# Nine expert blocks of the first two batches computed between the attention tiles of the last two, with a routing of their own

## The reference, cut to what matters

```python
# q, k, v: (4, 8, 576, 64); d_model 512; 8 experts, hidden size 1024
scores = q @ k.T / 8;  keep the 32 largest of each row;  softmax;  attn = p @ v
x = attn, heads side by side                                   # (4, 576, 512)
logits = x @ w_gate;  local = sigmoid(x @ w_local)
for b, s:                                                      # in order of s
    e = argmax(logits[b, s]) if s == 0 or local[b, s] < 0.5 else previous e
    p = softmax(logits[b, s])
    out[b, s] = p[e] * (relu(x[b, s] @ w1[e]) @ w2[e])         # a gated expert
X = real(fft(fft(out, axis=1), axis=2))
u = out + X;  result = u + relu(norm(u) @ w_ch1) @ w_ch2
```

## Time and profile before

| | us |
|---|---|
| median of 3 runs | 1572.55 (1571.76 to 1573.14) |
| the profiled execution | 1576.68 |
| its span, first to last instruction | 1574.9 |
| TensorE busy | 1410.1 (90%) |
| VectorE busy | 1075.2 (68%) |
| GpSimd busy | 635.8 (40%) |
| ScalarE busy | 605.1 (38%) |

### The profile page before, as it was taken

The page is one execution under the profiler, slowest core; times in us unless marked ns, Lnnn a source line. Parts: engine busy times, 40 slices in busy tenths (PEclk is TensorE's granted clock), DMA queues, the critical chain, the costliest instruction groups (busy, mean ns, idle before and its releaser), DMA issues. The chain is left out here.

```text
span 1574.9 us, 24676 instructions
## 1 busy us (share of the span) xinstructions
PE 1410.1 (90%) x8488; PEld 1205.7 (77%) x8488; DVE 1075.2 (68%) x2132; ACT 605.1 (38%) x1469; POOL 635.8 (40%) x520
## 2 busy tenths in 40 slices
PE   6888888888889889984889999968999999999998
PEld 5777777776767677773779999963678789989997
DVE  8999999999999999997435555546646422422222
ACT  3555545555555554541324444422322221321110
POOL 4666666666866666651344444332112100000000
PEclk9989989999899997995999999985899999999999
DMA  9101011111101110102142726443321111411111
GB/s 322 42 23 31 24 32 32 32 32 32 32 8 32 32 29 28 69 1 80 42 156 70 257 68 244 174 174 126 107 97 56 46 40 53 137 52 41 40 41 61
DMA packets 67938, 117.95 MB, mean 75 GB/s; under 512 B 27827, under 2 KB 27956, under 8 KB 67842
## 3 DMA queue, kind: packets, MB, share of 16 engines
q1 hardware_dynamic: 57306, 87.17, 16.9%
q0 software_dynamic: 9728, 28.06, 5.1%
q10 hardware_dynamic: 808, 1.48, 0.3%
HBM read 88.36 MB, written 31.99 MB: 76 GB/s over the span
## 5 line engine op out<-in xcount | busy, mean ns | idle before, releaser
L332 POOL TENSOR_SCALAR keep<-s_sb,top 128x576 f32<-128x576 f32 x142 | 244.8, 1724 | 223.7 <-DVE top L356 223.7
L356 DVE MAX8 top<-w_sb 128x8 f32<-128x576 f32 x432 | 303.9, 743 | 0.0
L227 PEld LDWEIGHTS ps_o<-v_sb,eT 128*128 128x128 f32 (+1 forms) x1440 | 197.5, 202 | 37.4 <-issue 26.3
L227 PE MATMUL ps_o<-v_sb,eT 128*128 128x74 f32 (+3 forms) x1440 | 221.5, 294 | 0.0
L1393 DVE SCALAR_TENSOR_TENSOR h_lo<-ps_ch,h_hi 128x384 fp32r<-128x384 f32 x96 | 53.5, 557 | 241.9 <-ACT h_hi L1244 241.8
L358 DVE MATCH_REPLACE8 w_sb<-top,w_sb 128x576 f32<-128x576 f32 x288 | 211.1, 739 | 0.0
L336 POOL TENSOR_TENSOR e_sb<-e_sb,keep 128x576 f32<-128x576 f32 x142 | 200.1, 1409 | 21.4 <-POOL keep L332 0.6
L199 PE MATMUL ps_t<-ident,e_sb 128*128 128x128 f32 x576 | 103.8, 307 | 97.3 <-POOL e_sb L336 91.3
L210 PE MATMUL ps_o<-ident 128*128 128x128 f32 x1152 | 174.5, 301 | 0.0
L789 PEld LDWEIGHTS ps_h<-bxT,w 128*128 128x128 f32 x1408 | 162.3, 194 | 5.6 <-DVEq L737 3.0
L789 PE MATMUL ps_h<-bxT,w 128*128 128x128 f32 x1408 | 163.1, 277 | 3.1 <-ACT bxT L833 3.1
(11 more groups left out here) (214 smaller groups left out, 2428.5 us busy)
## 6 DMA issues: line engine op xcount, KB each, us to landing
w<-in_w SPq DMA_DIRECT2D x18, 2048.0 KB, 13.2
stage<-in_w_ch SPq DMA_DIRECT2D x16, 512.0 KB, 3.8
q_sb<-in_q SPq DMA_DIRECT2D x16, 288.0 KB, 2.8
vT<-in_vt SPq DMA_DIRECT2D x16, 288.0 KB, 3.1
x_d<-rows SPq DMA_DIRECT2D x18, 256.0 KB, 2.4
u<-u_d SPq DMA_DIRECT2D x18, 256.0 KB, 2.8
x_d<-u POOLq DMA_DIRECT2D x18, 256.0 KB, 2.6
u<-x_d SPq DMA_DIRECT2D x18, 256.0 KB, 2.8
```

Source lines behind the costliest of these rows:

```text
L227: mm = pe.matmul(ps_o[k % 2][:, lo:hi], eT[k % NT_][0:n, c, :], v_sb[b][0:n, c, lo:hi], start=(c == 0), stop=(c == KC))
L332: pool.tensor_scalar(keep[t % 2][:, :], s_sb[t % NS][:, :], top[t % NS][:, TOPK - 1:TOPK], None, ALU.is_ge).then_inc(s_keep, 1)
L356: dve.max(eight, src).then_inc(s_top, 1)
```

## The change

In attention, steps t = 76 to 83 on, VectorE gets a second program (`early_routing`), a generator that is advanced twice after each top-32 instruction from pair 38 on. It computes the gates and the routing of the 1152 rows of batches 0 and 1, and the row numbers of the first NA = 9 blocks of their sorted list; TensorE's small matmuls for it stand in six steps (`HOPS`). From step 83 to 141 TensorE leaves out `keep_clock` and gets a list of 156 units instead, two or three in each step, in three places of it: per block one unit of four transposes, eight units of four fp32 matmuls (128 columns) and eight units of one fp32 matmul (512 columns), unsplit. ScalarE copies their results and issues the weight loads of each block (4 MB), GpSimd gathers and scatters. The rows that the nine blocks don't hold are routed with the 1152 rows of batches 2 and 3 in the second routing; the second expert stage goes through its used blocks alone, from both ends: six in a loop, three written out, 16 more each inside a test.

To free two PSUM banks, the scores of two tiles are computed in two halves in consecutive steps, with two copies of 288 columns for each tile in place of one of 576. GpSimd normalises two tiles a step from step 75. SyncE stores the first nine `x_d` tiles after the loads of head 10.

```diff
@@ attention @@
+    MIDDLE = NTILE // 2
+    ROUTE, NORM = MIDDLE // 2 + 2, MIDDLE + 3
+    HOPS = [(MIDDLE + n, at) for n, at in ((2, 2), (3, 2), (4, 1), (4, 2), (5, 2), (7, 2))]
+    AWAIT = [(ROUTE + n, at) for n, at in ((0, 9), (1, 0), (1, 7), (1, 10), (2, 0), (3, 1))]
-        ps_s = [pb(f"ps_s{n}", [P, 2, 512]) for n in range(2)]
+        ps_s = [pb(f"ps_s{n}", [P, 512]) for n in range(2)]
+        ps_a = [pb(f"ps_a{n}", [P, 512]) for n in range(2)]
+        UNITS = [("x", 0, 0)] + [("none", 0, 0)] * 3
+        for j in range(NA):
+            UNITS += [("h", j, m) for m in range(NF)] + [("y", j, m) for m in range(NF // 2)]
+            UNITS += [("x", j + 1, 0)] if j + 1 < NA else []
+            UNITS += [("y", j, m) for m in range(NF // 2, NF)]
+        EARLY0, EARLY1 = MIDDLE + 11, NTILE - 2
+        def units_at(t):
+            at = lambda x: min(max(len(UNITS) * (x - EARLY0) // (EARLY1 - EARLY0), 0), len(UNITS))
+            return UNITS[at(t):at(t + 1)]
@@ SyncE @@
-            for c in range(2):
-                load_w1(sp, env, (0, E - 1)[c], c)
-                load_w2(sp, env, (0, E - 1)[c], c)
+            def load_pair(i, b):
+                u = 2 * i + b
+                sp.wait_ge(s_qk, 2 * TPP * (u - 1) + 1 - b)
+                load_qk(u, b)
+                load_mid(u, b)
+                sp.wait_ge(s_vw, u - 1)
+                load_vt(u, b)
+                sp.wait_ge(s_pv, TPP * (u - 1))
+                load_v(u, b)
+            load_pair(NPAIR // 4 + 1, 0)
+            store_x(0)
+            load_pair(NPAIR // 4 + 1, 1)
@@ TensorE @@
+            def early_h(j, m, bank):
...
+                for k in range(KC):
+                    mm = pe.matmul(bank[:, (m % KC) * P:(m % KC + 1) * P], env["w1"][j % 2][:, k, m * P:(m + 1) * P],
+                                   a["xT"][:, k, :], start=(k == 0), stop=(k == KC - 1))
+            def early_y(j, m, bank):
...
+                mm = pe.matmul(bank[:, :], a["h"][:, m, :], env["w2"][j % 2][:, m, :], start=(m == 0), stop=(m == NF - 1))
+            def between(t, at):
...
+                for n, unit in enumerate(units_at(t)):
+                    if n % 3 == at:
+                        early(*unit)
                     turn(t)
-                    keep_clock(t)
-                if live(t + LQ) and (t + LQ) % 2 == 0:
-                    scores(t + LQ)
+                    if t < EARLY0:
+                        keep_clock(t)
+                    between(t, 0)
+                k = t + LQ
+                if live(k):
+                    scores(k - k % 2, k % 2)
+                between(t, 1)
                 if live(t - 1):
                     values(t - 1)
+                between(t, 2)
@@ ScalarE @@
+                    for n in (base, base + 1):
...
+                        act.activation(s_sb[n % NS][:, h * SH:(h + 1) * SH], ps_s[n % 2][:, 0:SH], ACT.Copy).then_inc(s_copy, 1)
+                if t == EARLY0 - 4:
+                    act.wait_ge(a["s_idx"], IDX_E)
+                    for j in range(2):
+                        early_w1(j)
+                        early_w2(j)
@@ GpSimd @@
+                for n in range(TPP):
+                    if t == NORM + n // 2:
+                        normalise(pool, ORDER[n], 0)
+                if t == EARLY0 - 1:
+                    pool.wait_ge(a["s_idx"], IDX_G)
+                    pool.wait_ge(env["s_xd"], 16 * HT)
+                    for j in range(2):
+                        gather(j)
+                for j in range(NA):
+                    if j + 2 < NA and t == unit_tile(("x", j, 0)) + 2:
+                        pool.wait_ge(a["s_t"], j + 1)
+                        gather(j + 2)
+                    if t == unit_tile(("y", j, NF - 1)) + 2:
+                        scatter(j)
@@ VectorE @@
                 for n in range(14):
                     top_op(c, n)
-                if c == NTILE // 4 + 2:
-                    dve.wait_ge(s_o, NTILE // 2)
-                    invert(slice(0, TPP), 0)
+                    now[0] = (c, n)
+                    if c >= ROUTE:
+                        next(routing, None)
+                        next(routing, None)
...
-            then(logits(slice(0, TPP), 0, 1))
@@ experts @@
+        SURE = NT - NA
+        def blocks(eng, used, body):
+            with eng.Fori(0, (SURE - 2) // 2) as i:
+                for c in range(2):
+                    body(i, c)
+            for j in range((SURE - 2) // 2 * 2, SURE):
+                body(j // 2, j % 2)
+            for j in range(SURE, NBLK):
+                with eng.If(used > j):
+                    body(j // 2, j % 2)
```

More of the change, by code:

```diff
@@ L88, in attention, with unit_tile @@
         s_norm = [sem(f"s_norm{b}") for b in range(2)]
+        s_rt = sem("s_rt")
+        r, a = choice_buffers(nc, ctx, "_a", ps_a), early_buffers(nc, ctx, env)
         block = ctx.enter_context(nc.Block(no_gpsimd_drain=True))
         LAST = NTILE - TPP
+        cst = env["cst"]
+        ones, below = cst[:, C_ONE:C_ONE + P], cst[:, C_UP:C_UP + P]
+        NF = F // P
+        UNITS = [("x", 0, 0)] + [("none", 0, 0)] * 3
[7 more added lines that the diff above has]
+            return UNITS[at(t):at(t + 1)]
+        def unit_tile(unit):
+            return next(t for t in range(EARLY0, EARLY1) if unit in units_at(t))
         @block.sync
@@ new lines, in store_x @@
+            def store_x(bb):
+                for m in range(TPP):
+                    rt = ORDER[m]
+                    n = bb * TPP + rt
+                    sp.wait_ge(s_norm[bb], m + 1)
+                    sp.dma_start(env["x_d"][n * P:(n + 1) * P, :], X[:, rt, bb * DM:(bb + 1) * DM]).then_inc(env["s_xd"], 16)
+            with sp.Fori(1, NPAIR // 4 + 1) as i:
+                for b in range(2):
+                    load_pair(i, b)
+            load_pair(NPAIR // 4 + 1, 0)
+            store_x(0)
@@ L158, in run, with normalise @@
+            load_pair(NPAIR // 4 + 1, 1)
+            with sp.Fori(NPAIR // 4 + 2, NPAIR // 2) as i:
+                for b in range(2):
+                    load_pair(i, b)
+            store_x(1)
+        def normalise(eng, rt, bb):
+            x = X[:, rt, bb * DM:(bb + 1) * DM].rearrange("p (h d) -> p h d", h=H)
+            eng.tensor_tensor(x, x, den[:, rt, H * bb:H * bb + H, None].broadcast_to([P, H, D]), ALU.mult).then_inc(s_norm[bb], 1)
         def run(body):
@@ L374, in _ @@
+            routing = early_routing()
             for c in range(NTILE // 2):
@@ L404, in _ @@
                     op.then_inc(env["s_lg"], 1)
-            for r in ORDER[early:]:
-                normalise(dve, r, 1)
+            for rt in ORDER[early:]:
+                normalise(dve, rt, 1)
 def wait_apart(eng, s, value, idle):
@@ L760, in load @@
                 renew(load_w2, s_w2)
-            with sp.Fori(0, LOOP) as i:
-                for c in range(2):
-                    load(i, c)
-            load(LOOP, 0)
-            for s in (s_w1, s_w2):
-                for c in range(2):
-                    sp.wait_ge(s[c], 16 * (LOOP + 2 - c))
+            blocks(sp, used_blocks(sp), load)
         @block.tensor
@@ L809, in _ @@
             turn(0, 0, 0)
-            def last(i):
-                return isinstance(i, int) and i == LOOP
+            used = used_blocks(pe)
             def body(i, c):
                 hidden(i, c)
-                if not last(i):
-                    turn(i, 1 - c, c + 1)
+                if_used(pe, used, i, c + 1, lambda: turn(i, 1 - c, c + 1))
                 output(i, c)
-            def skip(i, c):
-                j = 2 * i + c
-                passed(pe, s_h1, 2 * j + 4, 2)
-                turn(i, 1 - c, c + 1)
-                passed(pe, s_y, j + 2, 1)
-            blocks(pe, body, skip)
+            blocks(pe, used, body)
         @block.scalar
@@ L882, in _ @@
             dve.sem_inc(s_yf, 2)
-            blocks(dve, body, skip)
+            blocks(dve, used_blocks(dve), body)
         @block.gpsimd
```

585 lines of the change are left out of this document (397 added, 188 removed).

## The result

The changed kernel took 1610.46 us (median of four, 1602.82 to 1621.52) beside 1572.85 for the one before in the same group of runs: ratio 1.0241, 95% interval 1.0179 to 1.0304. It is slower, by 1.8 to 3.0%, where 1548 was forecast, and outside the range. The profiled execution is the fastest of its runs, 1602.82 (span 1601.0), against 1576.68 (1574.9).

A forecast was written before the change was run, and what follows sets the result against it. VectorE's top-32 search was taken to bound attention and TensorE the expert stage. Terms -95.7 + 14 + 12 + 42 + 3 + 1 - 0.5 = -24.2 turned 1572.55 into 1548 us, range 1518 to 1588.

The forecast's parts named there:

- How many blocks go: Expert stage: nine blocks bought early save six of 22 late, leaving 16 at 13.04 us; stage -95.7 us.
- rival (d): Expert stage: the nine early blocks save nine, so 13 remain, 3 × 13.04 less, 1509; chance 0.04.
- SyncE's order and GpSimd's wait: Near pair 43: stores queue behind head 10's v loads, gathers and mask behind the stores; +12 us, bounds 5 and 25.
- Early routing: VectorE in attention: 58 added instructions at 0.24 us each, all on the path; +14 us, bounds 6 and 20.
- TensorE from step 83 to 141: Attention beside the early units: TensorE becomes the bound, 5.53 us a tile against 4.82, 59 tiles; +42 us.
- The need by streams: TensorE, steps 83 to 141: 2.92 us a tile for attention plus 2.31 for early units, sum 5.23.
- The 0.30 a tile: TensorE, steps 83 to 141: allowance in us for changes of kind within a tile and the split scores.
- Rival (a): TensorE beside the early units: each mix of shapes costs a 0.34 us issue gap, tile 6.25, 84 for 42, 1591; chance 0.17.
- The tests: End of the expert stage: passed tests cost nothing, nine not taken partly hide in cover; +3 us, bounds 0 and 15.
- rival (c): End of the expert stage: each of nine skips costs 4.29 us, +29 in all, 1577; chance 0.08.
- Tail, second routing, first half: Attention's tail without keep_clock +1 us, second routing -0.5; no term for the stretch before pair 38.
- The sum -24.2: Whole kernel, in us: -95.7 + 14 + 12 + 42 + 3 + 1 - 0.5, a faster kernel.

The follow-up runs named there:

- the nested form: Second-stage block tests nested, against the kernel with six early blocks, own restart table, earlier stores and one routing instruction behind each search: 1524.01, ratio 0.9687.

## Why the prediction was wrong

**How many blocks go: the step that failed first.** "Together with the later 1152 they make 16 blocks" was counted with the reference's routing, not with the diff's table. The runs showed 18 blocks, and 16 once the table was mended (1152 and 1024 records). `C_SEG` is an 18-column table and the early scan has `HT * E` elements, nine for each expert. It cost 26 us; rival (d), that the change doesn't do what it says, had the right kind and the wrong sign. With 16 blocks the kernel took 1582.76, inside the range stated but still slower than before: this step alone doesn't make the forecast.

**SyncE's order and GpSimd's wait.** Place, mechanism and order were right, the term was mis-sized: 20.4 for 12. It took the stores' landing at 2.4 us as in the earlier trace rows and gave the weights in flight "a little", 1 us; beside them a store took 10.6, and without them the gap was 11.38. The result lies inside the bounds.

**Early routing.** 21.2 for 14, just above the bound of 20. Missing were 4.8 us of waits at the hops (2.13, 0.41, 2.22, where I had them 2 us ahead), 2.4 for the two instructions of `logits` (they left the end of attention, and the stretch from pair 71 to the first `hidden` got no shorter by it), and about 3 us in which small instructions stand still. That is more than the 7.2 that were missed; the rest of the 58 took about 0.19 each and not 0.24. VectorE's and GpSimd's timelines of the change:

```profile
409.75 0.17 DVE L732 TENSOR_SCALAR early_cnt<-ps_a 128x8 int32<-128x8 f32 x1 [2.22 <-PE ps_a L413]
409.95 0.46 DVE L733 TENSOR_SCALAR early_cnt<-early_cnt 128x8 int32<-128x8 int32 x1
...
425.04 1.32 DVE L766 TENSOR_SCALAR early_gidx<-early_tok 128x9 int32<-128x9 f32 x1
...
428.70 0.91 DVE L776 SCALAR_TENSOR_TENSOR early_mir<-early_tok,early_row 128x9 f32<-128x9 f32 x1
```

```profile
409.33 1.05 POOL L320 TENSOR_TENSOR rows<-rows,den 128x512 f32<-128x512 f32 x1
...
424.94 1.40 POOL L657 TENSOR_TENSOR e_sb<-e_sb,keep 128x576 f32<-128x576 f32 x1
...
428.18 1.41 POOL L657 TENSOR_TENSOR e_sb<-e_sb,keep 128x576 f32<-128x576 f32 x1
```

Most others on 8 or 9 columns take 0.14 to 0.20. The ones at 425.04 and 428.70 end with GpSimd's at 426.34 and 429.59, to 0.02 us, and three more (at 400.19, 409.95 and 413.25) end within some 0.03 us of a GpSimd instruction's end. All five stood beside a two-input `TENSOR_TENSOR` of GpSimd; L732, which reads PSUM (`ps_a`), took 0.17 beside the same one that held L733. The Trainium skill, Advanced Engine Details and Errata, section Mode Summary, has a rule: VectorE's second port is shared with GpSimd, so VectorE's instructions in a two-port mode and GpSimd's block each other. The trace agrees, with 0.2 to 1.15 us each time; one of the five (428.70) is a `SCALAR_TENSOR_TENSOR`, for which that section names no mode.

**TensorE from step 83 to 141.** 43.2 for 42, right by luck and for a wrong reason. The need by streams, 5.23 a tile, is what the chip took once nothing else stood in the way (5.25, 10.51 a pair, TensorE 100.00 of 100). The 0.30 a tile that I added for changes of kind did not show; in their place came 19 us of GpSimd's waits in front of masks. "GpSimd (3.1, plus about 0.5) stay below" looked at its load and not at its order. I had asked what queues behind the one wait for the stores, and not behind the gathers and scatters of every block. Rival (a), issue gaps, is out. The 0.34 us of the earlier trace rows were idle time of the weight load, and that costs nothing while matmuls still run: with GpSimd's order mended and TensorE's matmuls at 100.00 of 100, the same kind of wait is still there (waits of 500 to 700):

```profile
PEld ps_s L343 <- issue: 16.8, 29, 0.8
```

**The tests.** 3.6 for 3, for seven tests. By the count predicted, nine, it would have been 8.2 (13.69 against 5.51): the 3 came out by luck, since the wrong block count left seven. So rival (c) had something, at about 2 us a test and not 4.29. The Trainium skill's 0.11 us for a compare and branch (Advanced Engine Details and Errata, Control Flow Timing) is far below that; by its rule on fetches for taken branches (Runtime: NRT & Kernel Launch, Instruction fetch mechanics) each jump out of the window of instructions held waits for a fetch. No row shows a fetch: the 2 us a test leave room for one, and the nested form's single jump past eight blocks, 0.5 us at most, is either hidden or has none.

**Tail, second routing, first half.** +2.4 together for 0.5, and 2.7 in the mixer that was not looked into. That the split scores cost anything was no term at all, though the lead of the scores is in the diff; the 8 us that this part costs alone may be part of the difference between the profiled executions (26.1) and the medians (37.6), which is not shown.

The sum -24.2 thus missed by 50.3 in the profiled executions: 26.4 blocks, 8.4 landing, 7.2 routing, 8.3 the rest. By the medians it missed by 62; the 11.5 between the two are open.

## What to carry to other kernels

Count what a change saves with its own tables, not with the reference's. Work put beside other work needs room on every engine's queue as well as on its clock: for each in-order wait ask what stands behind it, and place it where what it waits for is long done. If a moved stage fills an engine, move less: six blocks gave 4%, nine 2.8.

## What was not expected of the hardware

- Nine stores of 256 KB landed after 10.6 us (median) beside 8 MB of loads, after 3.0 with the loads issued later, after 3.9 with the stores issued first, after 2.4 before.
- Four loads of 2 MB in a row kept ScalarE from its next instruction for 7.52 us in the change and 9.76 us where they were issued later.
- VectorE's small instructions stood still until a GpSimd `TENSOR_TENSOR` ended, up to 1.15 us, five times in one routing.
- Stretches at a granted clock of 0.50 with TensorE 10.00 of 10 busy lasted up to 40 us, and cost time where the scores' lead was short; before, none in attention lasted over 15.
- Blocks' tests that fail cost about 2 us each in a row behind some five that are hidden; nested, one jump past eight cost 0.5 us at most.
